# An attention and two MLPs on one core: the first two chunks reordered, the second tile's steps shifted

## The reference

```python
f = 1 / (1 + exp(-f_logit))
for t in range(S):
    state = f[:, :, t, :, None] * state + k[:, :, t] (outer) v[:, :, t]
    y[:, :, t] = q[:, :, t] @ state
x = y as [3072, 384]
xn = x / sqrt(mean(x * x) + 1e-6) * rms_g
x = (silu(xn @ w_gate) * (xn @ w_val)) @ w_out          # 1536 hidden
h = x @ w_in                                            # 2048 hidden
out = where(h >= 1, h, where(h <= -1, 0, (h + 1) ** 2 / 4)) @ w_out2
```

## Time and profile before

| | us |
|---|---|
| median of 3 runs (932.44 to 933.41) | 933.28 |
| the profiled execution | 932.01 |
| its span | 930.3 |
| TensorE busy | 920.9 |
| VectorE busy | 555.4 |
| ScalarE busy | 329.9 |
| TensorE's first matmul | 3.69 |
| first product of first_gate | 20.95 |

### The profile page before, as it was taken

How to read it: one execution, slowest core, us unless ns; L and a number is a source line. 1 busy time by engine, 2 the same in 40 slices (tenths; PEclk the granted TensorE clock), 3 DMA queues, 4 the chain that set the end, 5 groups by cost and what they waited for, 6 DMA issues and landing times.

```text
span 930.3 us, 18650 instructions
## 1 busy us (share of the span) xinstructions
PE 920.9 (99%) x7498; PEld 784.0 (84%) x7498; DVE 555.4 (60%) x975; ACT 329.9 (35%) x563; POOL 15.3 (2%) x35
## 2 busy tenths in 40 slices
PE   7999999999999999999999999999999999999998
PEld 4999999998888888888888888888888888888886
DVE  8987658757656575575555555445445545454453
ACT  4653333332223232332233434243333433433333
POOL 1000000000000000000000000000000000000000
PEclk9999999999999999999999999999999999999999
DMA  7822533532422442233313100000000000000000
GB/s 248 306 70 71 161 91 101 177 97 86 145 74 66 138 127 71 82 123 101 102 51 97 40 1 0 1 34 0 28 6 0 34 0 0 34 0 0 35 1 34
DMA packets 52276, 65.89 MB, mean 71 GB/s; under 512 B 14576, under 2 KB 42992, under 8 KB 52208
## 3 DMA queue, kind: packets, MB, share of 16 engines
q1 hardware_dynamic: 52064, 64.75, 21.9%
q10 hardware_dynamic: 144, 0.13, 0.0%
HBM read 51.43 MB, written 13.43 MB: 70 GB/s over the span
## 4 chain that ended last, share of the span: by engine, by line
PE 98%; DVE 1%; issue 1%; DMA 0%; ACT 0%; DVEq 0%
PE gate_ps L629 16%; PE val_ps L629 16%; PE acc L707 14%; PE acc L651 11%; PE gate_ps L695 11%; PE val_ps L695 11%; PE acc L711 7%; PE acc L655 5%; PE pair_ps L469 2%; PE y_ps L492 2%; PE y_ps L531 2%; PE pair_ps L520 1%; PE acc L722 0%; DVE after L1062 0%; DMA raw<-qkf_dram 0%
## 5 line engine op out<-in xcount | busy, mean ns | idle before, releaser
L993 ACT ACTIVATE raw<-raw,columns 128x512 f32<-128x512 f32 x96 | 69.4, 723 | 155.1 <-DVE raw L1453 155.1
L707 PE MATMUL acc<-high 128*128 128x512 f32 x282 | 109.7, 389 | 0.0
L707 PE MATMUL acc<-high,low 128*128 128x512 f32 x282 | 109.7, 389 | 0.0
L651 PE MATMUL acc<-high 128*128 128x512 f32 (+2 forms) x252 | 90.0, 361 | 0.0
L651 PE MATMUL acc<-high,low 128*128 128x512 f32 (+2 forms) x252 | 89.3, 358 | 0.0
L1000 ACT ACTIVATE high<-qd 128x512 fp32r<-128x512 f32 x96 | 60.7, 632 | 73.3 <-DVE qd L1458 73.3
L711 PE MATMUL acc<-low,high 128*128 128x512 f32 x282 | 79.2, 389 | 0.0
L1453 DVE TENSOR_SCALAR raw<-val_ps 128x512 f32<-128x512 f32 x48 | 33.2, 691 | 76.5 <-PE val_ps L695 76.5
L1453 DVE TENSOR_SCALAR raw<-gate_ps 128x512 f32<-128x512 f32 x48 | 33.1, 689 | 61.9 <-PE gate_ps L695 61.6
L1390 DVE TENSOR_TENSOR low<-qd,high 128x512 fp32r<-128x512 f32 x96 | 65.8, 685 | 5.7 <-ACT high L1000 5.1
L629 PE MATMUL gate_ps<-high 128*128 128x512 f32 (+2 forms) x249 | 65.0, 369 | 0.1
(11 more groups left out here) (153 smaller groups left out, 1698.8 us busy)
## 6 DMA issues: line engine op xcount, KB each, us to landing
raw<-qkf_dram SPq DMA_DIRECT2D x22, 770.0 KB, 4.8
x_all<-wb_dram SPq DMA_DIRECT2D x12, 576.0 KB, 6.7
kd_turn_dram<-after SPq DMA_DIRECT2D x19, 256.0 KB, 2.9
kd<-kd_turn_dram SPq DMA_DIRECT2D x76, 64.0 KB, 2.5
v_sb<-v_dram SPq DMA_DIRECT2D x23, 192.0 KB, 2.7
v_early<-v_dram SPq DMA_DIRECT2D x23, 192.0 KB, 2.6
out_dram<-x_all SPq DMA_DIRECT2D x5, 768.0 KB, 3.8
x_turn_dram<-x_all SPq DMA_DIRECT2D x19, 192.0 KB, 1.9
```

Source lines behind the costliest of these rows:

```text
L651: pe.matmul(acc[:, m, 0:width(i)], wb_part(w, j, 2, m), h_hi[:, j % 2, 0:width(i)], start=(j == 0 and w is w_hi), stop=False)
L707: pe.matmul(acc[:, m, 0:N2], wc_part(w, j, 1, m), h2_hi[:, j % 2, :], start=(j == 0 and w is w_hi), stop=False)
L993: nc.scalar.activation(act2_buf[:, j % 2, :], act2_buf[:, j % 2, :], ACT.Square, bias=half_col[:, :], scale=0.5).then_inc(square_ready, 1)
```

## The change

In words:
- The scores of chunks 0 and 1 go to banks of their own (first_scores), apart from the bank pair of the update products. attend(0) and attend(1) issue the update products first, then (for chunk 1 only) the products with the state, then wait for the mask. Chunk 0, whose state is zero, has no products with the state; VectorE clears y's bank instead.
- y of chunk 1 goes to gate_ps (second_y). Turned k, and x of chunk 0, go to val_ps; the three parts of chunk 1's x to the three banks of acc.
- turn_x(0) stands behind attend(1), and so do the rounding of chunk 0's x on ScalarE (behind the square sum of chunk 1) and its rest on VectorE. One keep_warm product is dropped.
- On VectorE decay_q(1) stands ahead of update_state(0), and mask_scores(1) ahead of normalise(0).
- Weight block 1 is loaded when the scores of chunk 1 are made, and so are the inputs of chunk 2; before, block 1 was loaded with block 0, and the inputs of chunk 2 once q of chunk 0 was made.
- sigmoid_f(2) and decay_after(2) move from the start into tile 0. All steps of the second tile come 3 slots later (DELAY), and a chunk follows the last by 8 slots instead of 9 (WINDOW).

```diff
-WINDOW = 9
+DELAY, WINDOW = 3, 8
...
-        turned_x = gate_ps
-        turned_parts = val_ps, acc[:, 1, :], acc[:, 2, :]
+        turned_parts = [acc[:, k, :] for k in range(KM)]
+        second_y = gate_ps[:, 0:DM + 1]
+        first_scores = acc[:, 1:3, 0:2 * UP].rearrange("s r (a t) -> s r a t", a=NP // 2)
+        second_squares = scores[:, :, :, :].rearrange("p r h t -> p (r h t)")[:, 0:DM + 1]
@@ SyncE @@
                 load_wb(0)
-                load_wb(1)
                 for part, x in enumerate(v_second):
                     sp.dma_start(x, v[1, :, 0, part * DM:(part + 1) * DM]).then_inc(v_second_loaded, 16)
-                sp.wait_ge(qd_ready, 1)
+                sp.wait_ge(scores_made, 2)
+                load_wb(1)
                 load_raw(2)
@@ TensorE, attend @@
-                    pe.wait_ge(scores_ready, n + 1)
+                    early_chunk = isinstance(n, int) and n < FIRST
+                    if not early_chunk:
+                        pe.wait_ge(scores_ready, n + 1)
...
-                    attend_state(n, c)
+                    if not early_chunk:
+                        attend_state(n, c)
                     for p in range(NP):
                         for b in range(NB):
                             mm = pe.matmul(update_ps[...], kdT[:, b, p, :], values[:, b // 2, p, :], ...)
                     mm.then_inc(update_made, 1)
+                    if early_chunk:
+                        if n > 0:
+                            attend_state(n, c)
+                        pe.wait_ge(scores_ready, n + 1)
@@ TensorE, first_attention @@
-                    turn_kd(0, acc[:, 1, :])
+                    turn_kd(0, val_ps)
                     score_alone(0, 0)
-                    keep_warm(WARM_SCORES)
                     attend(0, 0)
-                    turn_kd(1, acc[:, 1, :])
+                    turn_kd(1, val_ps)
                     score_alone(1, 1)
-                    turn_x(0, turned_x)
                     attend(1, 1)
+                    turn_x(0, val_ps)
                     keep_warm(WARM_LAST)
@@ all engines, second_tile @@
-                        o = slot - WINDOW * c
+                        o = slot - DELAY - WINDOW * c
@@ ScalarE, second_tile @@
+                        if o == 0 and c == 0:
+                            sigmoid_f(n)
@@ ScalarE, the start @@
                 split_wb(0)
-                round_x(0, 0, turned_x)
-                sigmoid_f(2)
                 square_sum(1)
+                round_x(0, 0, val_ps)
                 split_wb(1)
                 round_parts()
@@ VectorE, normalise_parts @@
                     dve.wait_ge(rstd_ready, 2)
+                    dve.wait_ge(xT_made, 1)
@@ VectorE, second_tile @@
-                        if o == 1 and c == 0:
-                            decay_k(n, c)
-                        elif o == 1:
+                        if o == (1 if c > 0 else 2):
                             decay_after(n, inputs)
-                        elif o == 3 and c > 0:
+                        elif o == (3 if c > 0 else 4):
                             decay_k(n, c, inputs)
@@ VectorE, the start @@
+                nc.vector.memset(y_ps[:, 0:DM], 0.0)
                 nc.vector.memset(y_ps[:, DM:DM + 1], (EPS * DM) ** 0.5)
+                nc.vector.memset(second_y[:, DM:DM + 1], (EPS * DM) ** 0.5)
...
                 decay_upto(1, 1, raw_second)
+                decay_q(1, 1, raw_second)
                 update_state(0)
-                decay_q(1, 1, raw_second)
                 decay_state(1, 1)
+                mask_scores(1)
                 dve.wait_ge(g_loaded, 16)
                 normalise(0)
-                mask_scores(1)
                 split_wb(0)
-                rest_x(0, 0, turned_x)
                 update_state(1)
-                decay_after(2)
+                rest_x(0, 0, val_ps)
                 normalise_parts()
```

More of the change, by code:

```diff
@@ L72 @@
 STAGE, STAGES = 3, 5
-WARM_START, WARM_SCORES, WARM_LAST = 2, 1, 2
+WARM_START, WARM_LAST = 2, 2
 AHEAD = 3
@@ L455, in score @@
                 def score(n, c):
+                    made = first_scores if isinstance(n, int) and n < FIRST else score_ps
                     for a in range(NP // 2):
@@ L463, in score @@
                                     rows = slice(r * HP, (r + 1) * HP)
-                                    to = score_ps[keys, r, a, :].rearrange("s (j t) -> s j t", t=HP)
+                                    to = made[keys, r, a, :].rearrange("s (j t) -> s j t", t=HP)
                                     if h == odd:
@@ L482, in score_alone, with outputs @@
                     score(n, c)
+                def outputs(n):
+                    return second_y[:, 0:DM].rearrange("t (r p e) -> t r p e", r=2, p=NP) if n == 1 else y_heads
                 def attend_state(n, c):
                     pe.wait_ge(wide_ready, n + 1)
-                    if n > 0:
+                    if n > 1:
                         pe.wait_ge(xs_ready, n)
@@ L491, in attend_state @@
                             q = slice(s * QW, (s + 1) * QW)
-                            pe.matmul(y_heads[q, :, p, :], qd[0:PR, half(n, c), p, q],
+                            pe.matmul(outputs(n)[q, :, p, :], qd[0:PR, half(n, c), p, q],
                                       wide[0:PR, p, :].rearrange("d (r e) -> d r e", r=2),
@@ L790, in square_sum @@
                     act.wait_ge(y_made, n + 1)
+                    if isinstance(n, int) and n == 1:
+                        act.wait_ge(xs_ready, 1)
+                        nc.scalar.activation(second_squares, second_y, ACT.Square, scale=DM ** -0.5, accum_out=ssq[:, :])\
+                            .then_inc(ssq_ready, 1)
+                        return
                     if isinstance(n, int) and n < CARRIED:
@@ L817, in second_tile @@
                         n = FIRST + c
-                        o = slot - WINDOW * c
-                        if o == 0 and c == 1:
+                        o = slot - DELAY - WINDOW * c
+                        if o == 0 and c == 0:
+                            sigmoid_f(n)
+                        elif o == 0 and c == 1:
                             sigmoid_f(n, raw_second)
@@ L1130, in mask_scores @@
                         dve.wait_ge(y_made, n)
-                    nc.vector.tensor_tensor(scores[:, :, :, :], score_ps,
+                    nc.vector.tensor_tensor(scores[:, :, :, :], first_scores if isinstance(n, int) and n < FIRST else score_ps,
                                             causal[:, :].unsqueeze(1).unsqueeze(1)
@@ L1149, in normalise_parts @@
                     dve.wait_ge(rstd_ready, 2)
+                    dve.wait_ge(xT_made, 1)
                     for k in range(KM):
                         columns = slice(k * P, (k + 1) * P)
-                        nc.vector.scalar_tensor_tensor(out=xs[:, columns], in0=y_ps[:, columns], scalar=rstd[:, :],
+                        nc.vector.scalar_tensor_tensor(out=xs[:, columns], in0=second_y[:, columns], scalar=rstd[:, :],
                                                        in1=g_rows[:, columns], op0=ALU.mult, op1=ALU.mult)\
```

8 lines of the change are left out of this document (4 added, 4 removed).

## The result

The changed kernel takes 936.21 us (median of 8 runs, 935.36 to 937.14), the kernel before 932.36 us in 8 runs of its own (931.94 to 933.41, the three above among them). The ratio is 1.0039, 95% interval 1.0030 to 1.0047: slower, by more than the 0.2% that can be told. The profiled executions took 936.56 and 932.01 us, their spans are 934.9 and 930.3.

The account below looks back on a forecast made before the run. VectorE and TensorE were taken as level in the reordered stretch of tile 0; start -0.55 and tile 0 +2.8 sum to +2.25 us, on 933.28 giving 935.5 us, range 932.9 to 937.3.

Parts of the forecast that it names:

- The start: Up to the first gate product: chunk 1 ready earlier, held by weight block 1's landing; -0.55 us (-1.4 to +0.3).
- tile 0: Where the second tile's chunks 2 to 4 are prepared: work and waits ahead of q(4) cost +2.8 us (+1.6 to +3.8).
- rivals 3 and 4: Block 1 lands late, sum +3.7 us, chance 0.12; TensorE falls to its lower clock, +2 us more, chance 0.06.
- The order of the slots: VectorE in tile 0: decay_after(2) ahead of q(4), +1.15 us, and q(4) one slot later, +2.06 us.
- wait at mask(3): VectorE in tile 0: chunk 3's mask, two steps behind q(3), must wait for scores; 0.6 us of new idle time.
- Split 2: VectorE in tile 0 waits because block 2, queued behind block 1 and chunk 2's inputs, lands late: 0.4 us (0 to 0.8).
- TensorE has its old work less gate 9: After the scores of chunk 4: only gate product 9, 1.08 us, is gone, and nothing VectorE owes is late.
- Rival 5: The 0.51 us issue gap at 17.05 us moves; inside dense tile 0 work it costs up to 0.5; no chance given.
- the gain stays: Rival: VectorE catches up in tile 0, only the start's -0.55 or -1.4 us remains, 931.9 to 932.7; chance 0.15.
- block 1 doesn't bind: Rival: block 1 lands by 18.0 us, start gives its full -1.4, sum +1.4, 934.7 us; chance 0.12.
- Block 1 was not late: Denies the rival that block 1 lands 5.5 us after issue: start +0.85, sum +3.7, 936.9 us; chance 0.12.
- The lower clock: Rival: TensorE's clock rises later or falls, 3 to 4 us of tile 0's products slow, +2 more, 937.5; chance 0.06.

Follow-up runs that it names:

- e9: The changed kernel run again without an edit: 935.92 us, one run.
- e1: The changed kernel with the second tile's old spacing (DELAY 0, WINDOW 9): 935.49 us, ratio 1.0031 to the kernel before.
- e6: The changed kernel with weight block 2 issued right behind block 1, ahead of chunk 2's inputs: 934.89 us, ratio 1.0029.
- e10: The kernel before run again without an edit: 932.25 us, one run.
- e2: The kernel before with only the new steps (DELAY 3, WINDOW 8), start and loads as before: 934.86 us, ratio 1.0027.
- e7: e3 with the second tile's old spacing (DELAY 0, WINDOW 9) and decay_after(2) in slot 1: 933.53 us, ratio 1.0013.
- e3: The changed kernel with weight block 1 loaded right behind block 0 again: 934.24 us, ratio 1.0020.
- e5: e2 with sigmoid_f(2) and decay_after(2) moved from the start into tile 0: 935.42 us, ratio 1.0039.
- e4: e3 with weight block 2 also loaded early, ahead of SyncE's wait for the scores of chunk 1: 934.94 us, ratio 1.0025.
- e8: e7 with block 2 issued ahead of chunk 2's inputs and sigmoid_f(2) and decay_after(2) in slot 2: 933.31 us, ratio 1.0015.
- e11: e7 run again without an edit: 932.93 us, one run.
- e12: e7 with the dropped warm-up product back behind the scores of chunk 0: 933.06 us, ratio 1.0010.

## Why the prediction was right, and where its sizes were off

Slower was forecast with 0.62 and came; 936.21 lies in the range 932.9 to 937.3. The difference was put at +2.25 us; the medians differ by 3.85 and the profiled executions by 4.55 (936.56 is 0.35 above its median, 932.01 is 0.35 below). That 935.5 came within 0.7 us of 936.21 owes 0.9 us to the first median of before, 933.28, which eight runs put at 932.36; counted from there, the same forecast would have been 934.6 and the top of the range 936.4, just above what was measured.

The mechanism was right and its size was not. The start was forecast at -0.55 and tile 0 at +2.8 us with bounds of +1.6 to +3.8; from G to T pass 52.71 us instead of 47.71, +5.00 (+4.89 in e9), outside these bounds. The measured +3.85 also lies outside the forecast's own +1.2 to +3.3. The range of the whole held because it left room for rivals 3 and 4, neither of which came; in that part it was luck.

**The start: -0.55 forecast, -0.44 measured** (-0.98 and -1.10 in e9 and e1, which have the same start). The path was right: q to scores to mask with the products under it, block 1 binding ScalarE, the parts behind it. Scores of chunk 1 were forecast for 13.72 and come at 13.69 in e6; in the changed kernel's own profile they come at 14.28 because the scores of chunk 0 took 1.42 us, and block 1 moves along with them, issued at 15.27, landed after 3.9 us instead of 4.1. That is chance: e9 and e10 show it come and go in either kernel. It also makes -0.44 agree better with the forecast than it should: the four profiles of the old start have G at 22.83 to 23.14 us, the four of this new one (after, e1, e6, e9) at 21.73 to 22.39, some 1.0 us earlier on average.

By the Trainium skill (DMA: Bandwidth & Descriptors, Anatomy of one DMA — SWDGE (gpsimd) path) a block would have needed an estimated 3.3 us. That fit is for transfers that GpSimd issues; these are SyncE's, and took 3.9 us here, 3.7 in e9 and 4.0 in e6, and the block bound. The row of 4.6 us that the prediction took for an idle queue was not one: 192 KB issued at 36.02 us and landing 4.2 us later were still under way at 37.0.

**The order of the slots: right in kind and size.** VectorE's busy time from G to Q grew by 37.41 - 34.02 = 3.39 us, forecast 1.15 + 2.06 = 3.21. The wait at mask(3) is 0.54 (forecast 0.6); the spare time went as forecast, -0.31. e2 shows the slots' share alone (with the waits that the move opened), e7 the scan's (1.17 us from G to Q). The scores of chunk 4 wait 1.14 us for q. The forecast named the place, the sign, and "over 1 us". Of the waits of 0.3 to 0.6 us that it put before the scores of chunks 2 and 3, that of chunk 3 came (0.42) and that of chunk 2 did not.

**Split 2: the term that was mis-sized most.** Forecast 0.4 (0 to 0.8), measured 1.43, and 0.30 more at the value product just ahead. Three parts of the working were short at once. The three transfers took 8.5 us from the first issue (15.27 to 23.76; 14.87 to 23.38 in e9), not 8.0. ScalarE wanted the block 7.1 us after that issue (23.78 - 1.42 - 15.27), not 7.4. And the 0.6 us of 22.7 against 22.1 were cut to 0.4 as if VectorE had work to cover the rest; it had none, and its 1.43 equals ScalarE's 1.42. In e9 the wait is 1.59, so it is no accident of one profile. e6, with only the issue moved, takes 1.2 us back. The 0.30 us at the value product is the place where e2 has its 0.63: the prediction noted that chunk 2's k decay had moved away from there, but put no price on that place.

**"TensorE has its old work less gate 9": wrong by 0.6 us.** From the scores of chunk 4 to T pass 75.10 - 62.57 = 12.53 us; 13.01 less 1.08 would be 11.93. Rival 5 had this: the gap of 0.51 us at the start vanished and one of 0.26 (0.51 from start to start) appeared in a dense part, the y products of chunk 4. It was left in the range instead of the sum. That the gap is the whole 0.6 us shows where it is missing: e2, e3 and e5, with the same order of slots, take 11.94, 11.95 and 11.93 us from these scores to T. Of the profiles with the new start's code nearly all have it (0.25 to 0.53 us idle in after, e1, e4, e6, e7, e8, e11, e12; in e9 one group of products takes 0.48 instead of 0.25 there), e3 alone does not, with the same TensorE program. Those with the old start's code (before, e10, e2, e5) have theirs in the state products of chunk 1 instead (0.20 to 0.73 us) and none at y of chunk 4. e4 has both.

The terms as measured, from the profile after: 3.39 + 1.43 + 0.30 + 0.54 + 0.13 (small rest) - 0.31 - 1.08 + 0.60 = 5.00 us, and 5.00 - 0.44 = 4.56.

**The rivals.** That the gain stays fell: 5.8 us more pass from G to Q. That block 1 doesn't bind fell in the changed kernel (0.89 us of ScalarE's idle time) and e3 shows what it would have been, a start of -1.52 us. Block 1 was not late. The lower clock did not take part in the profile after, whose windows show 1.00; two of its eight runs have 0.998, at 936.33 and 936.53 us, near the median. That it can take part at this place e1 shows.

## What to carry to other kernels

Where two engines are level in a stretch, a step moved into it costs its full time (less what falls into idle time that is there anyway, as in e5) and a later slot costs everything that then stands ahead of it, whatever the engine's share over the whole span says; a few microseconds of idle time at the start are the cheaper place for such work. When steps are moved later, look at what waits they filled (0.63 us in e2). For each transfer that is moved take the time of its own issue, and what is queued ahead of it, before its landing is put down as hidden. When products are taken out or moved, a gap put down to issue belongs into the sum, at the place where its count of instructions now falls, and not into the range.

## What was not expected of the hardware

**Gaps of TensorE that the trace puts down to issue keep to a count of instructions**: 0.20 to 0.80 us, always in runs of 32 to 48 small products. In all four profiles with the old start's code the gap stands behind the first 217 products and 218 weight loads that the trace records. In eight profiles with the new start's code one stands behind 970 products and 971 weight loads, though it falls at 62.6 to 67.7 us, in orders of the slots that differ, and in e12 with one product more ahead of it; the slow group of e9 is at that count too, and e3 alone has none. e4's gap of 0.80 us stands behind 219 and 219, nearly where the old start has its own. The size scatters when a kernel runs again (0.51 and 0.20 in before and e10, 0.31 and 0.51 in e7 and e11). The Trainium skill (Runtime: NRT & Kernel Launch, Instruction fetch mechanics) says that an engine's code is fetched in blocks of 256 instructions over a DMA queue of the sequencer's own, and that crossing into the next is mostly hidden. A place that keeps to the count and a size that scatters would agree with the first half; 0.2 to 0.8 us in a TensorE without slack is not hidden. The counts tie the gap to a place in the code and not to an operation or a time; that it is code fetch is argued, no run here isolates it.

**The clock can fall after a short wait inside dense work.** After 1.56 us of waiting in e1 TensorE ran at a granted 0.58 for 4.1 us. Within one kernel the runs with a mean clock of 0.998 are mostly longer: 935.56 against 934.66 in e1 (medians), 933.63 against 932.97 in e7, and the one such run of 25 of the kernel before is its slowest, 934.09. In e6, without that wait, all seven runs have 1.000. But the wait is not the whole condition: e3 and e4, whose profiles have no wait over 0.42 us between G and the scores of chunk 4, have two runs of ten each at 0.997 or 0.998, and e4's two (935.03 and 934.99) are no slower than its others. Where the clock fell in those runs no trace shows.

**The rate of the first score products is a matter of chance**: 0.95 or up to 1.43 us for the same 32 products at 8.7 us, in the same kernel, with nothing changed. The granted clock of that window reads 1.00 both times, as it also does for the first warm-up products at half rate, so only the durations tell.

**A queue delays the block behind it**: in the kernel after, 576 KB took 3.9 us as the first of the queue, and 6.5 us when issued 2.0 us behind it and 1.6 behind 770 KB; in e9 3.7 and 6.5.
